# Attention, expert routing and feed-forward in one kernel: parts of a batch's work trade places on VectorE and TensorE

## What is computed

```python
k_p = k.reshape(B, H, Sp, pool, D).mean(axis=3)          # B=8, H=8, S=576, D=64, pool=8: 72 keys
v_p = v.reshape(B, H, Sp, pool, D).mean(axis=3)
attn = softmax(q @ k_p.T / sqrt(D)); x = attn @ v_p      # (4608, 512), heads side by side
noisy = x @ w_gate + log1p(exp(x @ w_noise)) * noise     # 8 experts
# the two largest of each token, softmax over the two, each token through both experts
out[token] += weight * (relu(x[token] @ w1[e]) @ w2[e])
h = out @ w_in; result = (h - tanh(h)) @ w_out
```

## Time and profile before

| what | us |
|---|---|
| the three runs | 2058.49, 2059.75, 2053.21 |
| their median and mean | 2058.49, 2057.15 |
| the profiled execution | 2054.5 |
| its span, first to last instruction | 2052.8 |
| attention, period of one batch in the middle | 37.4 |
| mean granted TensorE clock over the span | 0.962 |

### The profile page before, as it was taken

The page is one execution under the profiler, slowest core; times in us unless marked ns, Lnnn a source line. Parts: engine busy times, 40 slices in busy tenths (PEclk is TensorE's granted clock), DMA queues, the critical chain, the costliest instruction groups (busy, mean ns, idle before and its releaser), DMA issues.

```text
span 2052.8 us, 36413 instructions
## 1 busy us (share of the span) xinstructions
PE 1921.9 (94%) x13088; PEld 1750.4 (85%) x13089; DVE 1035.7 (50%) x1987; ACT 821.7 (40%) x1720; POOL 581.7 (28%) x599
## 2 busy tenths in 40 slices
PE   7778863999999999999999988999999999999999
PEld 6777763989899999999998977899998899999888
DVE  4777774223131313132222326667777666777765
ACT  5655652223231323132222224444444444444444
POOL 4465553121211221122112122223222222222222
PEclk9888885999999999999999998999999999999999
DMA  8544413313131313132122312011000001000000
GB/s 237 139 125 128 117 47 120 109 62 123 61 123 41 133 51 123 41 112 72 61 103 65 119 61 83 32 54 38 31 31 31 31 31 61 31 31 31 31 31 21
DMA packets 75874, 152.31 MB, mean 74 GB/s; under 512 B 12640, under 2 KB 37344, under 8 KB 73024
## 3 DMA queue, kind: packets, MB, share of 16 engines
q1 hardware_dynamic: 59520, 108.42, 17.1%
q0 software_dynamic: 16320, 43.45, 6.4%
HBM read 111.51 MB, written 40.33 MB: 74 GB/s over the span
## 4 chain that ended last, share of the span: by engine, by line
PE 87%; DVE 6%; issue 3%; ACT 2%; DMA 1%; POOL 1%; DVEq 0%; ACTq 0%; POOLq 0%; SPq 0%
PE banks L728 13%; PE banks L727 13%; PE banks L726 13%; PE banks L717 13%; PE banks L718 12%; PE banks L719 12%; PE banks L621 3%; PE banks L707 3%; PE banks L600 2%; DVE k_raw L1030 1%; POOL slot_row L477 1%; PE banks L609 1%; PE banks L587 1%; DVE mx L1041 1%; ACT pr L843 1%
## 5 line engine op out<-in xcount | busy, mean ns | idle before, releaser
L717 PE MATMUL banks<-x_hi,w_hi 128*128 128x256 f32 x2304 | 638.6, 277 | 5.2 <-DVE x_lo L1224 4.1
L718 PE MATMUL banks<-x_lo,w_hi 128*128 128x256 f32 x2304 | 638.0, 277 | 0.0
L719 PE MATMUL banks<-x_hi,w_lo 128*128 128x256 f32 x2304 | 637.9, 277 | 0.0
L726 PE MATMUL banks<-w_hi,h_hi 128*128 128x512 f32 x1184 | 467.1, 395 | 3.0 <-DVE h_lo L1248 3.0
L728 PE MATMUL banks<-w_hi,h_lo 128*128 128x512 f32 x1184 | 466.1, 394 | 0.0
L727 PE MATMUL banks<-w_lo,h_hi 128*128 128x512 f32 x1184 | 463.0, 391 | 0.0
L717 PEld LDWEIGHTS banks<-x_hi,w_hi 128*128 128x128 f32 x2304 | 434.5, 189 | 8.2 <-DVE x_lo L1224 4.9
L718 PEld LDWEIGHTS banks<-x_lo,w_hi 128*128 128x128 f32 x2304 | 434.5, 189 | 2.5
L719 PEld LDWEIGHTS banks<-x_hi,w_lo 128*128 128x128 f32 x2304 | 434.4, 189 | 0.0
L563 POOL TENSOR_SCALAR large<-u_sq 128x512 uint8<-128x512 f32 x144 | 222.4, 1544 | 585.0 <-ACT u_sq L977 317.9
L1231 DVE SCALAR_TENSOR_TENSOR h_lo<-banks,h_hi 128x512 fp32r<-128x512 f32 x144 | 99.6, 692 | 379.0 <-ACT h_hi L928 379.0
(11 more groups left out here) (139 smaller groups left out, 2188.0 us busy)
## 6 DMA issues: line engine op xcount, KB each, us to landing
w_raw<-in_moe_w SPq DMA_DIRECT2D x32, 1024.0 KB, 5.2
y<-y_rows SPq DMA_DIRECT2D x18, 1024.0 KB, 5.0
k_raw<-in_k SPq DMA_DIRECT2D x16, 576.0 KB, 5.0
q_sb<-in_q SPq DMA_DIRECT2D x32, 288.0 KB, 3.5
v_raw<-in_v SPq DMA_DIRECT2D x16, 576.0 KB
x_rows<-x_sb SPq DMA_DIRECT2D x32, 288.0 KB, 3.5
out_x<-y_sb SPq DMA_DIRECT2D x36, 256.0 KB, 2.1
w_raw<-in_moe_w_in SPq DMA_DIRECT2D x4, 1024.0 KB, 4.8
```

The source lines that it names most:

```text
L717: pe.matmul(part, hi, x_hi[:, c, :], start=(c == 0), stop=False)
L718: pe.matmul(part, hi, x_lo[:, c, :], start=False, stop=False)
L719: mm = pe.matmul(part, lo, x_hi[:, c, :], start=False, stop=(c == NC - 1))
L726: pe.matmul(p_y[m][:, :], hi, w_hi[par][:, o:o + DM], start=(j == 0), stop=False)
```

## The change

`pool_keys(b + 1, 0)` goes from step 5 to step 4 on DVE, `part3` from step 4 to step 5, and `part4` from step 6 to step 7, where it stands ahead of `part5`. On PE `positions(b - 1)` goes from step 5 to step 6, behind `keys(b + 1, 0)`. In `X_ORDER` the counts (`cs`) stand behind the keys (`k0`) accordingly. ACT, POOL and SP have the same programs as before, but for the values of the counts that they wait for.

```diff
-        X_ORDER = [("vb0", 0), ("k1", 0), ("va1", 0), ("vb1", 0), ("cs", -1), ("k0", 1), ("va0", 1)]
+        X_ORDER = [("vb0", 0), ("k1", 0), ("va1", 0), ("vb1", 0), ("k0", 1), ("cs", -1), ("va0", 1)]
...
-            return b * len(X_ORDER) + (len(X_FIRST) - len(X_ORDER) + X_ORDER.index((name, of)))
+            n = X_ORDER.index((name, of))
+            if is_last(b) and name == "cs":
+                n -= 1
+            return b * len(X_ORDER) + (len(X_FIRST) - len(X_ORDER) + n)
...
-            return 0 if is_first(b) else b * len(X_ORDER) + (len(X_FIRST) - len(X_ORDER) - 2)
+            if isinstance(b, int) and b < 2:
+                return 6 * b
+            return b * len(X_ORDER) + (len(X_FIRST) - len(X_ORDER) - 3)
...
-                    if s == 5 and not first:
-                        positions(b - 1, x_use(b, "cs", -1))
                     if s == 6 and not is_last(b):
                         keys(b + 1, 0, x_use(b, "k0", 1))
+                    if s == 6 and not first:
+                        positions(b - 1, x_use(b, "cs", -1))
...
-                    if s == 5 and not is_last(b):
+                    if s == 4 and not is_last(b):
                         pool_keys(b + 1, 0)
...
-                        if s == 4:
+                        if s == 5:
                             part3(b - 1)
-                        if s == 6:
+                        if s == 7:
                             part4(b - 1)
                         if s == 7:
                             part5(b - 1)
```

## The result

| what | before | changed |
|---|---|---|
| median of 20 runs each | 2058.16 us (2052.79 to 2059.75) | 2066.84 us (2057.07 to 2072.24) |
| ratio of the times | | 1.0043, 95% interval 1.0032 to 1.0054 |
| profiled execution, its span | 2054.5, 2052.8 | 2060.76, 2059.0 |
| start of batch 1, of batch 7 | 46.5, 270.0 | 44.5, 274.1 |
| first scatter of the last batch's `part5` | 298.33 | 303.53 |

The changed kernel is slower by 8.7 us, 0.4%. The forecast was 2061: the time is inside the range, but just on the slower side of the bound of 0.3%, and I had 0.58 on "same" and 0.23 on "slower". The change itself is more than twice the +3.9 us of the forecast. Two things stand out: the profiled execution is 6.2 us longer than that of before, less than the medians say, and the runs of the changed kernel spread over 15 us where those of before spread over 7.

What follows compares the result with a forecast made beforehand. No engine fills a middle batch; PE's step 6 wait for DVE's `base` was the target. Batches 1 to 6 +3.0, first -1.0, last +1.9: +3.9 us, 2058.4 profiled, 2061 on the runs' level; range 2047 to 2070.

Steps and rivals of the forecast that it cites:

- rival (C): Turn between batches: clock stays at 0.50 where it rose before; 1.2 us a batch, +11 in all, 2068; chance 0.20.
- first batch: Batch without routing, only the sums of keys move: -1.0 us, bounds 0 and -3.
- last batch: `part3` ahead of `largest` of step 6 costs 1.1 us, `part4` ahead of `part5` 0.86: +1.9, bounds +0.9 and +2.0.
- my signs of being wrong: `part3` taking 1.8 us in step 5, PE's step 6 wait under 2 us, or step 7's clock no longer 0.50.
- `part3` in step 5 gives the gain back: DVE, step 5: POOL's sums hold the masks and their sum; 0.2 us is left of 2.3 gained.
- Rival (B): Step 5: the cast is held too; 0.2 us a batch, up to 0.6, +5 to +7, 2063; chance 0.07.
- The wait moves from `base` to `kT`: PE, step 6: `positions` waits for ACT's copy of the keys; idle 3.5 us, `scores` of head 7 0.4 us later.
- The turn: End of step 7 into the next batch: `values_cols` waits for `base`, 1.1 us later; +0.5 us for each of six batches.
- landing wait: DVE, `part5` in step 7: 0.75 us waiting for the scatter's landing, forecast to go, against 0.86 of added `part4`.
- (A): Step 5: short masks of `part3` are not held; 2.0 us a batch better than forecast, 2049; chance 0.15.
- (D): Step 6: the change doesn't decouple PE at all; in part the forecast itself, given no separate chance.
- (E): First batch and clock fall well, the middle costs nothing: -3 and less, about 2053 and below; chance 0.08.

Runs made afterwards that it cites:

- The fourth run: Changed kernel with POOL's value sums of heads 4 to 7 moved behind the scatter of the second choice: 2058.43 us, ratio 1.0005 to before.
- The first run: Changed kernel with `part4` back in step 6, all else as changed: 2050.28 us, ratio 0.9962 to before.
- the first series: Follow-up runs with edits to the changed kernel, timed where the kernel before took 2057.67 us.
- the third series: Changed kernel unedited and three other kernels side by side, where before took 2123.89 us; the changed kernel took 2125.20 us, ratio 1.0010.
- With the sums late, the changed order with `part4` back: Changed kernel with `part4` back in step 6 and POOL's value sums of heads 4 to 7 behind the second choice's scatter: 2112.51 us, ratio 0.9948.
- the old order with the sums late: Kernel before with POOL's value sums of heads 4 to 7 behind the second choice's scatter: 2106.54 us (0.9913), repeated at 2103.70 us (0.9899).

## Why the prediction was right, and where it was not

**The frame was right,** and the time is in the range because the range reached to rival (C) and beyond: measured was +6.2 us between the profiled executions and +8.7 between the medians, for a forecast of +3.9. The profiled execution is 6.2 us longer than that of before, forecast +3.9: first batch -2.0 (forecast -1.0, bounds 0 and -3), batches 1 to 6 +6.1 (forecast +3.0), last batch up to its first scatter +1.1 (forecast +1.9), and +1.0 behind it, where I had 0 and whose cause stays open. Most of what was to be seen was seen: sums of keys 1.53 and 0.55 in step 4, one mask of each pair over 1 us, PE's long wait in front of `tri` and ended by `kT`, `values_cols` waiting for `base`. But one of my signs of being wrong was there too: the granted clock over step 7 is no longer 0.50, but 0.69 to 0.78, though the `values` of head 5 still take 2.10 us.

**`part3` in step 5 gives the gain back:** right, from `rden` to `largest` 0.42 us is saved, where I had 0.2 and at most 0.5. The fourth run shows that POOL is the cause, 0.20, 0.44 and 0.20 us once it sums elsewhere. Rival (B) was half right: the cast is held (0.53 to 0.64 us in batches 2 to 6), but the sum doesn't end higher, since the first mask then runs free and `msum` waits for the same last instruction of POOL. This cast has a single input in SBUF, so the second half of what the Trainium skill says (GPSIMD Engine Reference, Key points), that instructions in a 2-port mode contend too, is the half that the trace agrees with, if the cast is one; the rows don't show its mode.

**The wait moves from `base` to `kT`:** right in place and size (3.38 to 3.61 us).

**The turn** is the step that failed, and with it the sentence ahead of it, "So I leave the clock as it is, at 0.50 behind it". The wait of `values_cols` for `base` came as I had it (1.10 to 1.27 us for 1.1). But I let the clock rise at 195.9, behind the `scores` of head 0, took the `values` of head 6 at 1.25 us and booked +0.5. In all six batches of the profiled execution it rose earlier, ahead of `values_cols`, so that these (0.41 us for 0.68) and the `scores` (0.97 for 1.68) ran at full clock. In batches 2, 4, 5 and 6 that makes good for the wait: in the second the first `rden` of the next batch comes 17.1 us behind that of step 5 (121.59 and 104.46), as before (196.57 and 179.48), and not 0.5 later. In batch 1, where the clock over step 7 had been 0.81 before and is 0.69 now, it comes 2.0 us later (17.6 for 15.6). The six are 3.3 us longer without batch 4's 2.8, 0.55 each on the mean, but the five others run from 0.3 to 1.3; that the mean is so near my 0.5 is in part luck.

At one turn of six the clock fell again, and the `values` took 2.07 us; by the estimate above that is about three of six in an ordinary run. It is the effect of rival (C), to which I gave 0.20, in a part of the batches, and at a higher price: I had 1.2 us for such a batch, measured was 2.8, since the step behind the turn is slow too. The way to it is another than (C)'s, though: the low stretch behind step 6 did not become longer than 10 us, it became shorter, and a second one followed. I treated the clock as having one outcome for the whole kernel. By my own numbers it rose at 195.9 and the `values` that hung on it were to start at 195.95; a term so close to an edge should have gone into the sum at a share. Three of six batches at the measured price are 8.4 us, which with the forecast is 2069. What makes the clock fall again at one turn and not at the next stays open.

**`part4` was mis-sized by its cover.** I charged 0.86 us of DVE against a landing wait of 0.75 and had the rest of the change at nothing. The first run shows the true parts: from batch 1 to 7 the rest of the change gains 3.7 us and `part4` in step 7 costs 9.8, 1.6 a batch with the second fall of the clock and 1.2 without. The landing wait of `row_id` did go, but what counts is PE, which had next to no spare time in step 7 before (busy for 8.67 of 8.70 us), while DVE had spare time in step 6 for all of `part4`: 1.65 and 1.20 us of idle. I had looked at what `part4` would meet in step 7 and never asked what it would have met in step 6 of the new order.

**Last batch:** `part3` in front of `largest` cost its 1.1 us; the 0.86 of `part4` were not seen. With `part4` in step 6 the first scatter is 29.6 us behind the batch's start, with it in step 7 29.4, so there its place makes no difference.

**Rivals.** (A) fell in what it was worth, not in its mechanism: one mask of two did find a gap of POOL's, in five of six batches, but only because the cast had been held to that gap, and the end of `part3` stayed where it was. (D) was right as far as my forecast took it in. (E) had the first batch right alone.

## What to carry to other kernels

When a step is moved, price both places in the new order: how long the engine is idle where it would have stood, and who waits where it now stands. With a new wait of about 1 us on TensorE at the turn the clock rose and fell elsewhere than before: at four turns of six that made good for the wait, at one it fell a second time and the batch behind it was 2.8 us longer. Such a term belongs in the sum at a share of the batches, not at its better value. And a hold between VectorE and GpSimd is not removed by moving one of them unless the place that it moves to has been looked at: here it went from the keys to the masks, and from the masks to `part4`.

## What the runs showed of the hardware

**A short cast is held like a sum.** The cast of 12 indices (one input, 96x12) takes 0.17 us alone and 0.53 to 0.64 beside POOL's sums; six elements of `wt` take 0.54 in place of 0.16.

**A second level of the chip.** Between the first series and the other two the kernel before became 66 us longer, and the changed kernel, timed on both levels, 58 us (2066.84 and 2125.20). The changed kernel was profiled on both. The first two batches are alike (31.1 and 38.5 us, here 32.1 and 38.6); from batch 2 on a batch takes about 47.7 us in place of 37.7, and 49.7 of the 62.8 us between the spans (2121.8 and 2059.0) are there when batch 7 begins (323.8 against 274.1). Batch 2 is the first with scatters of routing rows. Busy time of batch 4, two of the waits from 80 to 320 us (total, times, longest), and lines from the timeline of batch 5, of the changed kernel in the third series:

```profile
181.20:228.90 47.70, 32.81 (x255) 30.99 (x255) 28.54 (x93) 21.71 (x74) 20.98 (x24) 0.75 0.39 99
```
```profile
DVE rden L1053 <- remote: 18.3, 6, 3.4
ACT vT L853 <- remote: 16.0, 5, 3.3
```
```profile
242.37 1.25 PE L626 MATMUL banks<-vp,pT 128*96 128x81 f32 x12 [1.75 <-ACT pT L840]
243.95 0.41 PE L636 MATMUL banks<-ident,vp 72*64 72x72 f32 x4
246.27 0.92 POOL L482 DMA_INDIRECT slot_row<-row_id,slot_i  x1 [0.31 <-issue]
248.78 0.40 ACT L853 ACTIVATE vT<-banks 64x288 f32<-64x288 f32 x1 [3.18 <-remote]
249.77 2.21 PE L626 MATMUL banks<-vp,pT 128*96 128x81 f32 x12 [4.40 <-ACT pT L840]
```

ACT, DVE and POOL do the same work in nearly the same time (21.7, 28.5 and 21.0 us a batch, against 21.6, 27.7 and 21.0). What is new are waits for which the profile names no engine ("remote"), of up to 3.4 us, for results of PE: its transposes for `vT` are recorded from 243.95 on, 0.41 us, and ACT goes on at 248.78, 1.6 us behind the end of POOL's last scatter at 247.19. On the first level the same copy waited for nothing. The later `values` are slow besides (2.21 us), and the clock over a batch falls from 0.86 to 0.75. So some of PE's results reach the other engines about 3 us late, in stretches in which POOL scatters; that the scatters are the cause is not shown. PE's ends are modelled, so it can't be read whether PE itself was held or its signal, nor what sets the level; no run here tried it.

Only before and the changed kernel were timed on both levels, so it isn't shown that the kernels rank otherwise on this one. But such waits can decide between them here. With the sums late, the changed order with `part4` back has a wait of up to 7.4 us in front of `positions`, since the copy to `kT` is itself released late; its waits, and those of the old order with the sums late:

```profile
PE banks L653 <- ACT kT L826: 38.9, 6, 7.4
ACT kT L826 <- remote: 23.9, 5, 4.8
```
```profile
ACT kT L821 <- remote: 20.9, 5, 4.5
PE banks L578 <- DVE base L1134: 12.3, 5, 3.9
```

In the old order PE's one long wait of step 6 is 12.3 us in all, in place of 38.9.
